# Attention followed by two mixture layers on one core: where ScalarE copies the third turned tile in odd attention steps

## The reference

```python
def _attn_ref(q, k, v, s):                 # q, k, v: (4, 8, 576, 64); s: (4, 8, 576)
    scores = 1/sqrt(64) * q @ k^T
    cum = cumsum(maximum(s, 0))
    bias = -(cum[:, :, :, None] - cum[:, :, None, :])
    scores = where(causal, -1e9, scores + minimum(bias, 0))
    attn = exp(scores - max(scores))
    attn = attn / (sum(attn) + 1e-9)
    return attn @ v

x = attn_out as (2304, 512)
x = moe(x)       # 8 experts, the best 2 of each row, hidden 1024, relu
out = (sigmoid(x @ w_gate) * (x @ w_val)) @ w_out      # hidden 1536
```

## Time and profile before

| what | value |
| --- | --- |
| runs, median | 1274.19 us (1273.27 to 1275.47, 3 runs) |
| the profiled execution's own time | 1277.16 us |
| its span, first to last instruction | 1275.4 us |
| TensorE busy over the span | 1237.4 us (97%) |
| ScalarE busy | 512.6 us (40%) |
| VectorE busy | 497.1 us (39%) |
| GpSimd busy | 361.6 us (28%) |

### The profile page before, as it was taken

How to read it: one execution, slowest core, us unless ns; L and a number is a source line. 1 busy time by engine, 2 the same in 40 slices (tenths; PEclk the granted TensorE clock), 3 DMA queues, 4 the chain that set the end, 5 groups by cost and what they waited for, 6 DMA issues and landing times.

```text
span 1275.4 us, 23476 instructions
## 1 busy us (share of the span) xinstructions
PE 1237.4 (97%) x7362; PEld 1073.5 (84%) x7363; DVE 497.1 (39%) x924; ACT 512.6 (40%) x1184; POOL 361.6 (28%) x410
## 2 busy tenths in 40 slices
PE   8999999779999999999999999899999999999998
PEld 7777877478888888888888888799999999999997
DVE  7788886825060606050505080522231221313211
ACT  5888887743334343333433333412122121221211
POOL 4224541024443545453444463301010100100000
PEclk9999999689999999999999999999999999999999
DMA  4723232343242664233332411302010100100000
GB/s 101 203 62 77 65 69 78 108 134 100 65 148 82 214 199 146 92 122 105 109 124 90 148 33 42 116 2 71 4 51 25 42 34 0 49 25 0 25 1 25
DMA packets 100414, 101.57 MB, mean 80 GB/s; under 512 B 70196, under 2 KB 70196, under 8 KB 100336
## 3 DMA queue, kind: packets, MB, share of 16 engines
q1 hardware_dynamic: 82832, 64.06, 17.0%
q0 software_dynamic: 7280, 20.86, 5.9%
q10 hardware_dynamic: 10256, 16.06, 3.6%
HBM read 80.05 MB, written 22.73 MB: 81 GB/s over the span
## 4 chain that ended last, share of the span: by engine, by line
PE 86%; DVE 6%; issue 3%; ACT 3%; DMA 1%; DVEq 0%; ACTq 0%; POOL 0%; POOLq 0%
PE PB L1591 10%; PE PB L1590 10%; PE PB L1589 10%; PE PD L1589 9%; PE PD L1591 9%; PE PD L1590 9%; PE PA L1591 4%; PE PA L1589 4%; PE PA L1590 4%; PE PC L1440 3%; PE PC L1624 3%; ACT xtok L913 2%; DVE probT L1069 2%; PE PB L1486 2%; DVE Q L1059 2%
## 5 line engine op out<-in xcount | busy, mean ns | idle before, releaser
L1287 DVE CAST WX<-raw 128x1024 fp32r<-128x1024 f32 x56 | 56.4, 1007 | 278.0 <-DMA raw<-in_moe_w 278.0
L1330 DVE TENSOR_TENSOR gv<-sig,PB 128x384 f32<-128x384 f32 x72 | 39.9, 555 | 296.5 <-PE PB L1591 286.9
L757 POOL TENSOR_TENSOR hsTl<-hsT,hsTh 128x512 fp32r<-128x512 f32 x84 | 122.2, 1476 | 113.7 <-ACT hsT L968 113.7
L1589 PE MATMUL PB<-WX,xsTh 128*128 x344 | 138.0, 401 | 1.8 <-POOL xsTl L748 1.8
L1591 PE MATMUL PB<-WX,xsTl 128*128 x344 | 135.5, 394 | 0.0
L1589 PE MATMUL PD<-WX,hsTh 128*128 x336 | 135.2, 402 | 0.2 <-issue 0.2
L1590 PE MATMUL PB<-WX,xsTh 128*128 x344 | 135.3, 393 | 0.0
L1591 PE MATMUL PD<-WX,hsTl 128*128 x336 | 131.6, 392 | 0.0
L1590 PE MATMUL PD<-WX,hsTh 128*128 x336 | 130.9, 390 | 0.0
L1006 ACT ACTIVATE sig<-PA 128x384 f32<-128x384 f32 x72 | 35.4, 492 | 184.4 <-PE PA L1591 184.4
L1011 ACT ACTIVATE gvh<-gv 128x384 fp32r<-128x384 f32 x72 | 37.8, 525 | 160.2 <-DVE gv L1330 160.2
(11 more groups left out here) (246 smaller groups left out, 2664.9 us busy)
## 6 DMA issues: line engine op xcount, KB each, us to landing
raw<-in_moe_w SPq DMA_DIRECT2D x28, 1024.0 KB, 5.2
y_d<-ys ACTq DMA_DIRECT2D x43, 256.0 KB
out<-fin SPq DMA_DIRECT2D x18, 256.0 KB, 2.1
qin<-in_q SPq DMA_DIRECT2D x32, 128.0 KB, 2.4
vin<-in_v SPq DMA_DIRECT2D x32, 128.0 KB, 2.4
raw<-in_moe_w ACTq DMA_DIRECT2D x4, 1024.0 KB
x_d<-xtok SPq DMA_DIRECT2D x16, 256.0 KB, 2.0
kin<-in_k SPq DMA_DIRECT2D x28, 128.0 KB, 2.4
```

The lines of the kernel that those rows point to most:

```text
L757: nc.gpsimd.tensor_tensor(hsTl[:, cols], hsT[:, cols], hsTh[:, cols].bitcast(F32), ALU.subtract).then_inc(hTl_done, 1)
L1287: nc.vector.tensor_copy(high, source).then_inc(w_high, 1)
L1330: nc.vector.tensor_tensor(gv[:, :], sig[:, :], PB[:, 512 * (f % 2):512 * (f % 2) + GN], ALU.mult).then_inc(gv_done, 1)
L1589: pe.matmul(acc, hi, w_hi, start=first, stop=False)
```

## The change

In ScalarE's order of an odd step, `copy(2)` is put ahead of `high(0)`. Nothing else is changed.

```diff
                 else:
                     exp(0)
                     copy(0)
                     exp(1)
                     copy(1)
                     exp(2)
+                    copy(2)
                     high(0)
-                    copy(2)
                     high(1)
                     exp(3)
                     exp(4)
```

## The result

The changed kernel took 1282.45 us (median of 6 runs, 1278.27 to 1285.42), the kernel before 1274.96 us in the runs beside it. The ratio is 1.0058, with a 95% interval of 1.0038 to 1.0078: slower by 7.4 us, with 4.8 to 9.9 as the bounds. The profiled execution was one of 1282.29 us with a span of 1280.5, 5.1 us over the span of before.

A forecast was written before the change was run, and what follows sets the result against it. Attention was bound by a circle of waits from ScalarE's high part of k through VectorE and TensorE, 12.87 us. Fifteen odd steps at 0.49 us add 7.3 to the 1274.19 median: 1281.5 us, range 1280.0 to 1283.5 (8 in 10: 1278.5 to 1286.5).

The forecast's parts named there:

- (e): TensorE, odd step: the 0.32 us wait before the fifth tile's turning goes, worth nothing; its wait for VectorE's copies becomes 1.15.
- (a): ScalarE, odd step: the first high part of k starts later by the moved third tile's copy, 0.49 us.
- my lower bound of 6.9: Lower outer bound of the added time in us: 15 odd steps at the copy's busy time of 0.46 us.
- (b): Moved copy on ScalarE: its transposes are done 0.16 us before it, so no wait; 0.1 us allowed where cover is missing.
- (c): ScalarE's second high part starts when it did; its low part and GpSimd's copy of the second half stay hidden.
- (d): VectorE's low parts, minimum and two turned tiles move by 0.49 us; ScalarE's 0.96 us wait absorbs its later last exponential.
- (f): Other queues: SP's loads move with the steps, and early expert weight copies are not the last to arrive; no cost.
- TensorE's wait decides: Rival: losing TensorE's 0.32 us wait before the fifth tile's turning gains 4.8 us over 15 steps, giving 1269.4; chance 0.04.
- Absorption: Rival: other waits in the steps take up part of the delay, leaving 0.17 us each, 1276.8 us; chance 0.09.
- The clock: Rival: longer waits before the 15 turnings drop TensorE's clock; four more falls give 1287.1 us, all some 1300; chance 0.15.

## Why the prediction was right, and where it was not

**The sign and the mechanism.** Right, with one thing missed, of which (e) tells. The row that was to decide, VectorE's wait for the first high part in each odd step, did: the wait grew in all 15 steps, VectorE ran without a gap behind it, and TensorE's turning waited for its copies. The period grew by 0.35 us, and extra work of 0.20 us behind the third tile's copy in the changed kernel added 0.18 more. All three numbers of the profile were forecast too large: a period of 13.36 us (from one first high part to the next, as here from one first low part) and measured 13.23, 17.7 us of VectorE's idle time and 16.0, a span of 1282.7 and 1280.5. The reason is (a), and for the span the clock as well.

**(a) The size of the term.** Too large: 0.49 us forecast, 0.37 measured (116.09 to 116.46). I took the time from the copy's start to the next instruction's start in the order of before, and the next instruction was the second high part. That one starts later behind whatever stands ahead of it: in the kernel before 0.03 us after the copy's end (112.78 against 112.75), where the first high part in the changed kernel starts 0.10 before the end of the copy. From the third tile's or the first high part's start to the exponential behind them ScalarE takes 1.57 us before (111.76 to 113.33) and 1.58 after (116.09 to 117.67). So the other 0.12 us go with the second high part, not with the copy. So the sum should have been 15 x 0.37 = 5.6 us and not 7.3, which lies under my lower bound of 6.9. The estimate of 0.62 from the Trainium skill (ScalarE: Activation LUTs, Rules for kernel authors) is further off, and not for the page's fault: its 0.3 us is for an activation whose bias is a pointer operand. The exponentials have such a bias, and the third one, of the same 128x384, takes 0.62 us (115.48); the copy has none and takes 0.47.

**(b) Cover for the moved copy.** Right: it starts without a wait behind the exponential, at 116.09, while the transposes began at 115.43. The 0.1 us that I allowed for steps without that cover wasn't needed: VectorE's wait for the first high part grows by 0.37 to 0.38 us in 14 of the 15 steps, and by 0.52 in the other, where the wait of before was 0.19 us shorter than usual.

**(c), (d)** Right in their order. ScalarE's last exponential now waits 0.27 us and ends in time, since ScalarE's wait before the next step's first copy is the same 0.96 us.

**(e) TensorE has 0.34 us to spare.** This step was wrong, though it didn't change the forecast. The wait for the fifth tile's turning did go, and TensorE did wait longer for VectorE's copies, by 0.62 us before 120.11; with the 0.34 inside the three transposes (0.83 less 0.49) that is 0.96 where I had 1.15. But I took the first copies as the only thing that TensorE could be late for. The second score tile was due at the same time for VectorE's second minimum, and the order of before has both chains even: delaying only the copy by 0.20 us cost 0.20 in the period, by 0.79 us 0.81. The change lengthened one chain and shortened the other; only the first counts.

**(f) Other queues.** Nothing on them was late through the change. But I overlooked the four loads on ScalarE's own queue behind step 5. They move by the same amount as the step does, so they add nothing to the change's cost; but one of them that happens to be slow can add 0.7 us and more to an execution of either order.

**The total.** My 7.3 us of difference met 7.4 of the ratio, but partly by chance. The steps show 5.9: 0.37 in the first and 5.5 in the 14 periods. About 0.7 of that is the slow load, which leaves 5.2 us for the change, within the interval of 4.8 to 9.9. The changed kernel with split loads, at 1.0043 or 5.5 us, agrees. For the rest of the median's difference I have no cause that the runs show, other than that falls of the clock at the start and behind attention, and a slow load, come and go, and six runs don't even them out. The prediction also had the time from 210 us on unchanged; the profile has it 2.0 us shorter, 1.6 of them by the clock's fall in the profile of before.

**The rivals.** That TensorE's wait decides was nearer the truth than my 4% said, in that its wait was on the path, but it could not turn the sign: the rule of the Trainium skill (Perfetto Trace Analysis, Optimization Strategy), to make what blocks the most contended engine start sooner, moved the wait to another place on the same engine and added to it. Absorption didn't occur. The clock didn't fall in the steady steps: TensorE's longer wait, 0.62 us in one piece, left the granted clock at 1.00 from 30 to 200 us.

## What to carry to other kernels

Where an order written by hand is well balanced, a wait on one chain says only that this chain is not the last to have started, not that it has room: follow it to where it meets the other, and take the lag of the wait itself (here 0.39 us) into the account. Moving an instruction then lengthens one chain by all of it and gains nothing on the other. Starting both chains earlier took 0.10 us from the period, which the time hardly shows; a gain clear of the noise came only when what closed behind them, a shared buffer, was opened as well.

## What was not expected of the hardware

ScalarE's start-to-start times depend on the pair: the same copy of 128x384 takes 0.37 us ahead of the first high part and 0.49 ahead of the second, which reads partitions 64 to 127 and writes 0 to 63 where the first stays in its own. Whether the crossing of partitions is the cause was not tried. And a DMA issue of these loads on ScalarE's queue mostly takes 0.4 to 0.6 us, but in 11 of the 13 profiled executions at least one of the four took from 0.64 to 1.83; it matters where compute stands behind it on the same queue.
